# Attention rounds 9 to 17 woven into two expert steps, on one core

## Chip, cores and metric

The kernel runs on one core of a Trainium2 chip. The metric is the device time in microseconds (us) of one execution. Every comparison is with the kernel before.

## What is computed

```python
# attention in chunks of 64 tokens, 8 heads of 64, 2304 tokens in all
scores = scale * np.matmul(q_c, k_c.transpose(0, 1, 2, 4, 3))
scores = scores - np.max(scores, axis=-1, keepdims=True)
attn = np.exp(scores)
attn = attn / (np.sum(attn, axis=-1, keepdims=True) + 1e-09)
x = np.matmul(attn, v_c)                       # -> (2304, 512)
# mixture of 8 experts, each 512 -> 1024 -> 512
P = np.exp(x @ w_gate - max)                   # then 8 rounds of row and column scaling
out += P[:, e:e + 1] * (np.maximum(x @ w1[e], 0.0) @ w2[e])
# one dense layer, 512 -> 2048 -> 512, with elu between
y = elu(out @ w_in) @ w_out
```

Matrix products are done in three passes: each operand is split into a high part (rounded) and a low part (the rest), and high·high, low·high and high·low are added.

## The kernel before

**Tokens.** The 2304 tokens are 18 tiles of 128. Six blocks of three tiles form three *pairs* (p = 0, 1, 2) of 768 tokens. The attention visits the tiles pair by pair, one tile in each of 18 *rounds*, so pair 0 is complete after round 5, pair 1 after round 11, pair 2 after round 17.

**A round** `i` of the attention, on the engines: TensorE forms the scores (`scores_of`, L442, 32 recorded matmuls of 64 rows); VectorE takes the row maximum (L956) and subtracts it (L961); ScalarE does the exponential (L692); VectorE sums the row (L967), adds eps (L969) and takes the reciprocal (L973); GpSimd multiplies (`norm`, L311); TensorE transposes the probabilities (`turn_prob`, L453), ScalarE copies them out of PSUM (`e_copy`, L698), TensorE multiplies them with the values (`values_of`, L468), ScalarE copies the result to `x` (`x_copy`, L703). TensorE's order in round `i` is `scores_of(i)`, `turn_prob(i-3)`, `values_of(i-4)`. The value tile `v_wide` holds 64 rows of values and 64 rows of zeros for each half, so that a matmul can contract over all 128 rows. VectorE writes the zeros at the start.

**A step** `n` is one pair of tokens against one group of 256 hidden columns. It has seven *products* M1 to M7 of six matmuls of 384 columns each (`product`, L477; a scheme of Strassen's kind with 7 products for 8), and a *down* phase of 36 matmuls of 512 columns (L494 to L509) into the accumulators. There are 3 steps for each group, 32 groups of experts (steps 0 to 95) and 8 of the dense layer (steps 96 to 119, kind `elu`). Between a product and the down phase lie a copy on ScalarE (`fork`), an add on VectorE (`join`, L1009), the activation on ScalarE (`high`) and its low part on VectorE (`low`, L1014).

**The operands of the products** come from `x`: four sums on VectorE (`x_sums`, L991), seven high parts on ScalarE (`x_high`, L720), and seven low parts, on GpSimd (`x_low`, L364) or VectorE (L1002). Before a pair's first step TensorE waits for all of them at once (`x_split`).

**Order around the change.** Every engine runs a list written out by hand; semaphores join the lists. TensorE does rounds 0 to 17, then step 0 with what is left of the attention between its products, then the gate of the router for blocks 0 and 1 (`gate_of`, L582), step 1, more gates, step 2. From step 3 on the steps follow without a gap. SyncE issues all loads, in order, from one queue (`load_qk` of 512 KB and `load_v` of two times 128 KB for each round; four buffers each). A load waits for its buffer: `load_qk(i)` for the scores of round i-4, `load_v(i)` for the values of round i-4. What stands behind a waiting load waits too.

Steps 95 to 98 carry the second change of operands: the accumulators of the experts are transposed into `x`, and the operands for the dense layer are formed pair by pair.

## Time and profile before

| | |
|---|---|
| median of 3 runs | 1996.67 us (1993.13 to 1996.77) |
| the profiled execution's own time | 1995.51 us |
| its span in the trace | 1993.7 us |
| TensorE matmul busy | 1945.5 us, 98% |
| VectorE, ScalarE, GpSimd busy | 56%, 36%, 27% |
| mean granted TensorE clock | 0.993 |

The profile is one execution. Busy time of TensorE is a share of the span in which a matmul was in flight. The granted clock is 1.00 for 2.4 GHz and 0.50 for 1.2 GHz. Times in the trace count from the start of the span.

### The profile page before, as it was taken

The page shows a single profiled execution, that of the slowest core. Times are in us where ns is not written, and L with a number is a line of the kernel's source. Part 1 is how long each engine was busy: PE and PEld are TensorE (multiplying, and loading weights), DVE is VectorE, ACT ScalarE, POOL GpSimd, SP SyncE. Part 2 cuts the span into 40 slices and gives each one's busy share as a digit, 9 for nine tenths or more (in the row PEclk, how much of TensorE's full clock was granted, in tenths as well). Part 3 has the DMA queues.
Part 4 walks back from the last instruction along what each step waited for, and adds up shares of the span by engine and source line. Part 5 has one row for each costly group of instructions (what it writes and reads, how often), then busy time and mean ns, then how long its engine had stood idle before and what let it go on. Part 6 is the DMA issues. An engine that isn't in the chain of part 4 may idle for free.

```text
span 1993.7 us, 31492 instructions
## 1 busy us (share of the span) xinstructions
PE 1945.5 (98%) x10738; PEld 1751.2 (88%) x10738; DVE 1123.3 (56%) x1866; ACT 719.5 (36%) x1516; POOL 532.8 (27%) x600
## 2 busy tenths in 40 slices
PE   6799999999999999999999999999999989999999
PEld 5699999988999889998899988999889868998888
DVE  7766654555545555455554555555555576666666
ACT  4532223222233323232223322223323455555554
POOL 5732252222222222222222222222222342222220
PEclk9999999999999999999999999999999989999999
DMA  8110000000000000000000000000000000000002
GB/s 257 52 39 26 22 21 22 21 21 21 21 21 21 21 21 32 31 21 21 21 21 21 21 21 21 21 21 21 21 25 28 11 21 22 21 21 21 21 21 95
DMA packets 20154, 61.40 MB, mean 31 GB/s; under 512 B 2960, under 2 KB 2960, under 8 KB 20112
## 3 DMA queue, kind: packets, MB, share of 16 engines
q1 hardware_dynamic: 20112, 60.84, 9.0%
q8 instruction: 26, 0.43, 0.1%
q14 instruction: 16, 0.13, 0.0%
HBM read 56.12 MB, written 4.72 MB: 31 GB/s over the span
## 4 chain that ended last, share of the span: by engine, by line
PE 93%; DVE 4%; ACT 1%; issue 0%; POOL 0%; ACTq 0%
PE bank L477 44%; PE bank L507 5%; PE bank L494 5%; PE bank L495 5%; PE bank L509 5%; PE bank L508 5%; PE bank L499 5%; PE last_banks L507 3%; PE last_banks L509 3%; PE last_banks L508 3%; PE last_banks L494 3%; PE last_banks L495 3%; PE last_banks L499 3%; DVE x_sum L991 1%; ACT x_hi L720 1%
## 5 line engine op out<-in xcount | busy, mean ns | idle before, releaser
L477 PE MATMUL bank<-x_hi,w_hi 128*128 128x384 f32 x1680 | 568.5, 338 | 14.5 <-DVE x_lo L1002 6.9
L477 PE MATMUL bank<-x_hi,w_lo 128*128 128x384 f32 x1680 | 565.9, 337 | 0.0
L477 PE MATMUL bank<-x_lo,w_hi 128*128 128x384 f32 x1680 | 564.6, 336 | 0.0
L746 ACT ACTIVATE h_raw<-bank 128x384 f32<-128x384 f32 x360 | 176.6, 491 | 746.5 <-PE bank L477 744.7
L1009 DVE TENSOR_TENSOR h_raw<-bank,h_raw 128x384 f32<-128x384 f32 x360 | 200.7, 558 | 421.2 <-PE bank L477 419.6
L477 PEld LDWEIGHTS bank<-x_hi,w_hi 128*128 128x128 f32 x1680 | 316.6, 188 | 24.9 <-issue 7.8
L477 PEld LDWEIGHTS bank<-x_lo,w_hi 128*128 128x128 f32 x1680 | 316.6, 188 | 5.5
L319 POOL TENSOR_TENSOR w_sum<-raw 128x256 f32<-128x256 f32 x40 | 29.5, 739 | 1088.6 <-PE bank L477 1081.7
L477 PEld LDWEIGHTS bank<-x_hi,w_lo 128*128 128x128 f32 x1680 | 316.4, 188 | 0.0
L1027 DVE SCALAR_TENSOR_TENSOR acc<-bank,route,acc 128x512 f32<-128x512 f32 x336 | 240.4, 751 | 125.4 <-PE bank L509 125.4
L755 ACT ACTIVATE h_hi<-h_raw 128x384 fp32r<-128x384 f32 x288 | 151.2, 526 | 208.6 <-DVE h_raw L1009 208.6
L1027 DVE SCALAR_TENSOR_TENSOR acc<-last_banks,route,acc 128x512 f32<-128x512 f32 x168 | 120.2, 751 | 161.8 <-PE last_banks L509 161.8
L507 PE MATMUL bank<-w_hi,h_hi 128*128 128x512 f32 x480 | 188.4, 393 | 3.6 <-DVE h_lo L1014 3.6
L494 PE MATMUL bank<-w_hi,h_hi 128*128 128x512 f32 x480 | 189.3, 394 | 0.7 <-DVE acc L1021 0.7
L1014 DVE SCALAR_TENSOR_TENSOR h_lo<-h_raw,h_hi 128x384 fp32r<-128x384 f32 x288 | 179.8, 625 | 16.1 <-ACT h_hi L755 4.6
L495 PE MATMUL bank<-w_lo,h_hi 128*128 128x512 f32 x480 | 188.5, 393 | 0.0
L509 PE MATMUL bank<-w_hi,h_lo 128*128 128x512 f32 x480 | 187.5, 391 | 0.0
L508 PE MATMUL bank<-w_lo,h_hi 128*128 128x512 f32 x480 | 187.4, 390 | 0.0
L499 PE MATMUL bank<-w_hi,h_lo 128*128 128x512 f32 x480 | 149.2, 392 | 0.0
L347 POOL TENSOR_TENSOR w_lo<-raw,w_hi 128x512 fp32r<-128x512 f32 x80 | 103.8, 1303 | 46.6 <-ACT w_hi L736 44.9
L341 POOL TENSOR_TENSOR w_lo<-w_sum,w_hi 128x256 fp32r<-128x256 f32 x160 | 114.8, 739 | 0.0
L507 PEld LDWEIGHTS bank<-w_hi,h_hi 128*128 128x128 f32 x480 | 90.2, 188 | 25.4 <-DVE h_lo L1014 4.9
(103 smaller groups left out, 2561.0 us busy)
## 6 DMA issues: line engine op xcount, KB each, us to landing
raw<-in_w_up SPq DMA_DIRECT2D x40, 512.0 KB, 3.2
raw<-in_w_down SPq DMA_DIRECT2D x40, 512.0 KB, 3.3
qk<-in_q_k SPq DMA_DIRECT2D x18, 512.0 KB, 5.9
v_wide<-in_v SPq DMA_DIRECT2D x36, 128.0 KB, 3.6
out<-acc SPq DMA_DIRECT2D x18, 256.0 KB, 2.0
gate_w<-in_w_gate SPq DMA_DIRECT2D x1, 16.0 KB, 7.1
```

What stands on the lines that cost most here:

```text
L477: mm = nc.tensor.matmul(up_ps[s], w[:, s, kk, :], xs[:, s, kk, :], start=first and s in (M1, M2, M5), stop=kk == 1 and w is w1_lo, skip_gr ...
L494: nc.tensor.matmul(y_ps[i], h_hi[:, fi, ti, js], w2_hi[:, f, :], start=True, stop=False)
L495: nc.tensor.matmul(y_ps[i], h_hi[:, fi, ti, js], w2_lo[:, f, :], start=False, stop=False)
L499: nc.tensor.matmul(y_ps[TPB * h[1] + j], h_lo[:, fi, ti, js], w2_hi[:, f, :], start=False, stop=False)
L507: nc.tensor.matmul(y_ps[i], h_hi[:, fi, ti, js], w2_hi[:, f, :], start=False, stop=False)
L508: nc.tensor.matmul(y_ps[i], h_hi[:, fi, ti, js], w2_lo[:, f, :], start=False, stop=False)
L509: nc.tensor.matmul(y_ps[i], h_lo[:, fi, ti, js], w2_hi[:, f, :], start=False, stop=True)\
L746: nc.scalar.activation(h_raw[:, to[0], to[1], :], src, ACT.Copy).then_inc(fork_done, 1)
L755: nc.scalar.activation(h_hi[:, h[0], h[1], :], src, ACT.Relu).then_inc(h_hi_done, 1)
L1009: nc.vector.tensor_tensor(raw, src, raw, ALU.add).then_inc(join_done, 1)
L1014: nc.vector.scalar_tensor_tensor(h_lo[:, h[0], h[1], :], src, 0.0, h_hi[:, h[0], h[1], :].bitcast(F32), ALU.max, ALU.subtract).then_inc(h_ ...
L1027: nc.vector.scalar_tensor_tensor(acc[:, t, :], y_ps[i], route_flat[:, bass.ds(EXPERTS * t + expert, 1)], acc[:, t, :], ALU.mult, ALU.add). ...
```

## The change

1. The values tile has 64 rows per head half and no zeros; a values matmul contracts over 64 rows (`v_rows`). One load of 256 KB replaces two of 128 KB. The eight zero fills are gone.
2. `soft` has a 65th column that holds eps, so that the row sum includes it; the add of eps is gone. `norm` writes another tile, `prob`. Both have three buffers.
3. Rounds 0 to 8 use two sets of score banks in turn. Steps 0 and 1 are no longer behind the attention: round 9 goes with M1 of step 0, 10 with M2, and so on to round 14 with M7; rounds 15 to 17 and the last transposes and values go with the products of step 1. The values follow the transpose by one product, not by a round.
4. Low parts of the token sums of pairs 0 and 1 (M5, M6, M3, M7) are formed on VectorE, of pair 2 M6, M3, M7.
5. TensorE waits for the low part of each product before that product (`x_split(u, s)`), in the later pairs too.
6. SyncE's list of loads is written in another order; the loads of the first weights come earlier.
7. The gates, the conversion of the first weights, the scaling rounds of the router (one step later) and `scale_acc` move to fit.

```diff
-OVERLAP = {M1: 18, M5: 19, M3: 20, M7: 21}
-LOWS_POOL = [7, 14, 17, 22, 27, 32]
-LOWS_DVE = [0, 0, 4, 6, 8, 10]
+EARLY = 9
+ROUND_OF = {0: {M1: 9, M2: 10, M5: 11, M6: 12, M3: 13, M7: 14}, 1: {M2: 15, M5: 16, M6: 17, M3: 18, M7: 19, M4: 20}}
+LOWS_POOL = [[M1, M2, M4], [M1, M2, M4], [M1, M5, M2, M4]] + [[M1, M2, M4, M5, M7]] * 3
+LOWS_DVE = [[M5, M6, M3, M7], [M5, M6, M3, M7], [M6, M3, M7]] + [[M6, M3]] * 3
...
             load_qk(0)
             load_qk(1)
+            sp.dma_start(raw1[:, :, :], w_up[0, :, :, :]).then_inc(raw1_loaded, 16)
+            load_qk(2)
             load_v(0)
-            load_qk(2)
+            load_qk(3)
             load_v(1)
-            load_qk(3)
+            sp.dma_start(raw2[:, :, :], w_down[0, :, :, :]).then_inc(raw2_loaded, 16)
             load_v(2)
             load_v(3)
-            for i in range(TILES):
-                if i + DEPTH < TILES:
-                    load_qk(i + DEPTH)
-                if DEPTH <= i:
-                    load_v(i)
-                if i == 1:
+            for i in range(DEPTH, TILES):
+                load_qk(i)
+                load_v(i)
+                if i == 8:
                     sp.dma_start(gate_w[:, :, :], w_gate.rearrange("(k p) e -> p k e", p=P)).then_inc(gate_loaded, 16)
-                    sp.dma_start(raw1[:, :, :], w_up[0, :, :, :]).then_inc(raw1_loaded, 16)
-                    sp.dma_start(raw2[:, :, :], w_down[0, :, :, :]).then_inc(raw2_loaded, 16)
...
-            def x_split(u):
-                pe.wait_ge(x_lo_done, LOWS_POOL[u])
-                if LOWS_DVE[u] > 0:
-                    pe.wait_ge(x_lo_rest, LOWS_DVE[u])
+            def x_split(u, s):
+                if s in LOWS_POOL[u]:
+                    pe.wait_ge(x_lo_done, low_count(LOWS_POOL, u, s))
+                else:
+                    pe.wait_ge(x_lo_rest, low_count(LOWS_DVE, u, s))
...
+            for i in range(EARLY):
+                scores_of(i)
+                if i >= TURN_LAG:
+                    turn_prob(i - TURN_LAG)
+                if i > TURN_LAG:
+                    values_of(i - TURN_LAG - 1)
...
+                def ahead(s):
+                    i = ROUND_OF[n].get(s)
+                    if i is None:
+                        return
+                    if i < TILES:
+                        if n == 1:
+                            pe.wait_ge(acc_done, 5)
+                        scores_of(i)
+                    if i == EARLY:
+                        values_of(i - TURN_LAG - 1)
+                    turn_prob(i - TURN_LAG)
...
+                    i = ROUND_OF[n].get(s)
+                    if i is not None:
+                        if n == 1:
+                            pe.wait_ge(acc_done, 6)
+                        values_of(i - TURN_LAG)
...
-                dve.wait_ge(sum_done, 3 * i + 1)
-                nc.vector.tensor_scalar(row_den[:, :], row_sum[:, :], EPS, None, ALU.add).then_inc(sum_done, 1)
```

**Place one: SyncE's queue, the loads of rounds 4 to 7.** `qk_74` to `qk_77` are the four q and k buffers (rounds 4 to 7 reuse them in turn), `v_wide_78` to `v_wide_81` and `v_rows_78` to `v_rows_81` those of the values. Before, with the q and k of rounds 6 to 8 first and then the values of round 4:

```order
L260 DMA qk_76<-in_q_k 128x1024 [waits scores_done]
L260 DMA qk_77<-in_q_k 128x1024 [waits scores_done]
L260 DMA qk_74<-in_q_k 128x1024 [waits scores_done]
L268 DMA v_wide_78<-in_v 64x512 [waits values_done]
L268 DMA v_wide_78<-in_v 64x512
L260 DMA qk_75<-in_q_k 128x1024 [waits scores_done]
```

The same place in the change:

```order
L279 DMA v_rows_81<-in_v 128x512
L273 DMA qk_74<-in_q_k 128x1024 [waits scores_done]
L279 DMA v_rows_78<-in_v 128x512 [waits values_done]
L273 DMA qk_75<-in_q_k 128x1024 [waits scores_done]
L279 DMA v_rows_79<-in_v 128x512 [waits values_done]
L273 DMA qk_76<-in_q_k 128x1024 [waits scores_done]
```

Before, four loads of q and k (rounds 5 to 8) stood ahead of the first load that waits for values; now only that of round 4 does, and each later one stands behind the values load of the round before it.

**Place two: TensorE, round 5 of the change.** `first_banks` and `last_banks` are the two sets of score banks, `e_t` the transposed probabilities.

```order
L471 MATMUL first_banks<-qk_75 64x64 [waits soft_done,qk_loaded1]
L471 MATMUL first_banks<-qk_75 64x64 x15
L482 MATMUL bank<-ident,prob_87 128x128 [waits prob_done,e_t_done]
L482 MATMUL bank<-ident,prob_87 128x128 x3
L495 MATMUL bank<-e_t,v_rows_79 64x64 [waits e_t_done,v_loaded1]
L495 MATMUL bank<-e_t,v_rows_79 64x64 x15
L471 MATMUL last_banks<-qk_76 64x64 [waits soft_done,qk_loaded2]
```

The order within a round is that of before, with other names: the values of round 1 come behind the scores of round 5 and ahead of those of round 6.

**Place three: GpSimd, around the last low part of pair 0.** `x_lo_51` holds the low parts of pair 0, `x_lo_54` those of pair 1. Before, behind the sixth `norm` from the start of pair 0's low parts:

```order
L364 TENSOR_TENSOR x_lo_51<-x,x_hi_49 128x768 [waits x_hi_done]
L311 TENSOR_TENSOR soft_82<-soft_82,row_rec_97 128x512 [waits sum_done]
L364 TENSOR_TENSOR x_lo_51<-x,x_hi_49 128x768 [waits x_hi_done]
L311 TENSOR_TENSOR soft_83<-soft_83,row_rec_98 128x512 [waits sum_done]
L364 TENSOR_TENSOR x_lo_51<-x_sum_50,x_hi_49 128x768 [waits x_sum_done,x_hi_done]
```

In the change:

```order
L321 TENSOR_TENSOR prob_85<-soft_82,row_rec_98 128x512 [waits e_turned,sum_done]
L321 TENSOR_TENSOR prob_86<-soft_83,row_rec_99 128x512 [waits e_turned,sum_done]
L374 TENSOR_TENSOR x_lo_51<-x,x_hi_49 128x768 [waits x_hi_done]
L374 TENSOR_TENSOR x_lo_54<-x,x_hi_52 128x768 [waits x_hi_done]
L321 TENSOR_TENSOR prob_87<-soft_84,row_rec_98 128x512 [waits e_turned,sum_done]
```

GpSimd's low part of M4 of pair 0 (the first of the two `x_lo` rows) now stands behind the `norm` of round 13; before, one low part followed each `norm`.

## Rows read from the trace of the kernel before

**Rows 1.** Busy time by stretch, then granted clock, DMA share, GB/s.
```profile
0.00:10.00 10.00, 2.26 (x64) 1.92 (x64) 6.53 (x12) 1.91 (x2) 0.85 (x7) 1.00 0.84 265
10.00:20.00 10.00, 7.53 (x168) 6.35 (x168) 8.13 (x19) 3.49 (x6) 3.63 (x4) 1.00 1.05 352
71.72:98.17 26.45, 24.94 (x218) 21.21 (x218) 13.72 (x14) 13.55 (x23) 14.98 (x8) 0.90 0.01 2
98.17:141.57 43.40, 41.98 (x224) 37.86 (x224) 27.60 (x49) 15.12 (x32) 13.71 (x12) 1.00 0.07 25
141.57:157.29 15.72, 15.72 (x82) 14.29 (x81) 10.12 (x22) 4.58 (x10) 5.95 (x7) 1.00 0.20 68
1627.50:1633.30 5.80, 5.74 (x18) 5.77 (x19) 2.21 (x3) 1.01 (x2) 0.00 (x0) 0.50 0.00 0
```

**Rows 2.** TensorE in order of time, rounds 7 to 9.
```profile
30.47 1.12 PE L453 MATMUL bank<-ident,soft 128*128 128x128 f32 x4 [3.89 <-ACT e_t L698]
31.51 1.98 PE L468 MATMUL bank<-e_t,v_wide 128*64 128x64 f32 x32
33.42 1.13 PE L442 MATMUL last_banks<-qk 64*64 64x64 f32 x32
35.72 1.23 PE L468 MATMUL bank<-e_t,v_wide 128*64 128x64 f32 x32
36.88 0.69 PE L442 MATMUL last_banks<-qk 64*64 64x64 f32 x32
38.14 0.66 PE L453 MATMUL bank<-ident,soft 128*128 128x128 f32 x4 [0.56 <-ACT e_t L698]
```

**Rows 3.** SyncE's queue in order of time: start, duration of the issue.
```profile
36.99 1.10 SPq L268 DMA_DIRECT2D v_wide<-in_v  x2
```

**Rows 4.** Loads from issue to landing (last column), issued at 38.1 and 145.2.
```profile
qk<-in_q_k SPq DMA_DIRECT2D x1, 512.0 KB, 4.1
raw<-in_w_up SPq DMA_DIRECT2D x1, 512.0 KB, 3.3
```

**Rows 5.** VectorE in order of time, one round and one sum.
```profile
58.02 0.64 DVE L956 TENSOR_REDUCE row_max<-last_banks 128x8 f32<-128x512 f32 x1
58.69 0.69 DVE L961 TENSOR_TENSOR soft<-last_banks,row_max 128x512 f32<-128x512 f32 x1
59.30 0.68 DVE L967 TENSOR_REDUCE row_sum<-soft 128x8 f32<-128x512 f32 x1
60.01 1.02 DVE L969 TENSOR_SCALAR row_den<-row_sum 128x8 f32<-128x8 f32 x1
61.06 0.20 DVE L973 RECIPROCAL row_rec<-row_den 128x8 f32<-128x8 f32 x1
68.11 0.91 DVE L991 TENSOR_TENSOR x_sum<-x_sum,x 128x768 f32<-128x768 f32 x1
70.10 2.39 DVE L991 TENSOR_TENSOR x_sum<-x 128x768 f32<-128x768 f32 x1
```

**Rows 6.** GpSimd in order of time, the same stretches.
```profile
58.18 1.04 POOL L311 TENSOR_TENSOR soft<-soft,row_rec 128x512 f32<-128x512 f32 x1 [0.35 <-DVE row_rec L973]
59.18 1.82 POOL L364 TENSOR_TENSOR x_lo<-x_sum,x_hi 128x768 fp32r<-128x768 f32 x1
```

**Rows 7.** TensorE, VectorE, GpSimd at the entry of step 97, in order of time.
```profile
1627.56 0.66 PE L477 MATMUL bank<-x_hi,w_hi 128*128 128x384 f32 x1 [6.94 <-DVE x_lo L1002]
1622.41 5.01 DVE L1002 TENSOR_TENSOR x_lo<-x_sum,x_hi 128x768 fp32r<-128x768 f32 x2
1619.93 6.67 POOL L364 TENSOR_TENSOR x_lo<-x,x_hi 128x768 fp32r<-128x768 f32 x3 [2.22 <-ACT x_hi L720]
1631.78 0.56 DVE L1009 TENSOR_TENSOR h_raw<-bank,h_raw 128x384 f32<-128x384 f32 x1 [2.63 <-PE bank L477]
1636.55 0.39 PE L494 MATMUL bank<-w_hi,h_hi 128*128 128x512 f32 x1
```

**Rows 8.** The chain of work, two blocks of the gate: start, us.
```profile
122.61 2.80 PE last_banks L582 x16
```

More of the change, by code:

```diff
@@ L78, in nth_hidden, with low_count @@
     return HIDDEN[kind].index(h) + 1
+def low_count(lows, u, s):
+    return sum(len(lows[v]) for v in range(u)) + lows[u].index(s) + 1
 def pair_tile(p, i):
@@ L864, in _ @@
-            relu_step(0, begin=True, after=overlap)
-            for c in range(3, 7):
-                x_high(0, 1, c)
-            for c in range(3):
-                x_high(0, 2, c)
+                    x_high(0, M2)
+            x_copy(5)
+            e_copy(6)
+            exp_of(9)
+            fork(0, up_a, H11, M1, "first")
+            x_copy(6)
+            e_copy(7)
+            x_high(0, M5)
+            exp_of(10)
+            x_copy(7)
+            x_high(0, M6)
+            e_copy(8)
@@ new lines, in _ @@
+            exp_of(11)
+            x_high(0, M3)
+            fork(0, up_b, H22, M5, "first")
+            x_copy(8)
+            e_copy(9)
+            exp_of(12)
+            x_high(0, M7)
+            fork(0, up_a, H12, M6, "first")
+            x_copy(9)
+            high(0, H11, "first")
+            e_copy(10)
+            exp_of(13)
+            x_high(0, M4)
+            x_copy(10)
+            x_high(1, M1)
+            e_copy(11)
+            exp_of(14)
+            x_high(1, M2)
+            x_copy(11)
@@ L869, in _ @@
+            e_copy(12)
+            x_high(1, M3)
+            exp_of(15)
+            x_copy(12)
+            x_high(1, M7)
+            e_copy(13)
+            exp_of(16)
+            fork(1, up_b, H22, M5, "first")
+            x_copy(13)
+            high(1, H11, "first")
+            x_high(1, M4)
+            e_copy(14)
+            exp_of(17)
+            fork(1, up_a, H12, M6, "first")
+            x_copy(14)
+            e_copy(15)
+            x_copy(15)
             gate_copy(0)
             gate_copy(1)
[L872 to L878 removed]
@@ L1129, in _ @@
[L1129 to L1146 removed]
+            softmax_head(0)
@@ new lines, in _ @@
+            join(0, H11, up_c, M2, 1, "first")
+            softmax_head(13)
+            x_low(0, M7)
+            softmax_tail(12)
+            low(0, H11, "first")
+            softmax_head(14)
+            softmax_tail(13)
+            join(0, H12, up_b, M3, 3, "first")
+            join(0, H22, up_a, M7, 2, "first")
+            low(0, H12, "first")
+            low(0, H22, "first")
+            low(0, H21, "first")
+            softmax_tail(14)
+            x_sums(1, (M5,))
+            for i in range(TPB):
+                add_tile(0, 0, i, "first")
@@ new lines, in _ @@
+            x_sums(1, (M6,))
+            for i in range(TPB, 2 * TPB):
+                add_tile(0, 0, i, "first")
+            x_low(1, M5)
+            x_sums(1, (M3,))
+            softmax_head(15)
+            x_low(1, M6)
+            x_sums(1, (M7,))
+            softmax_head(16)
+            x_low(1, M3)
+            softmax_tail(15)
+            join(1, H11, up_c, M2, 1, "first")
+            softmax_head(17)
+            x_low(1, M7)
+            softmax_tail(16)
+            low(1, H11, "first")
@@ new lines, in _ @@
+            softmax_tail(17)
+            join(1, H12, up_b, M3, 3, "first")
+            join(1, H22, up_a, M7, 2, "first")
+            low(1, H12, "first")
+            low(1, H22, "first")
+            logits_of(0)
+            logits_of(1)
+            low(1, H21, "first")
+            x_sums(2, (M5, M6))
+            for i in range(TPB):
+                add_tile(1, 1, i, "first")
+            x_sums(2, (M3, M7))
+            for i in range(TPB, 2 * TPB):
+                add_tile(1, 1, i, "first")
```

517 lines of the change are left out of this document (265 added, 252 removed).

## The prediction, made before the changed kernel had run

> **What bounds the kernel now.** I read the busy time by stretch first [rows 1]. From 141.57 us, where step 3 begins, TensorE is busy without a gap: step 3 takes 15.72 us, all of it matmul, and the later steps are like it. So the change can move the time in two places only: ahead of step 3, and at the entry of the dense layer (steps 96 to 98), where the trace has TensorE's one long wait behind the start, 6.94 us [rows 7]. The time ahead of step 3 is what I work out, since everything behind it follows TensorE's work.
>
> Ahead of step 3 the attention runs almost alone until 71.72 us. Scores of round 9 start at 36.88 us [rows 2]; from there VectorE sets the pace, with 3.2 us or more for a round: in the one shown row maximum, subtraction, row sum, add of eps and reciprocal start at 58.02, 58.69, 59.30, 60.01 and 61.06 [rows 5]. The add of 8 numbers took 1.02 us because GpSimd held something VectorE needed: its low part ran from 59.18 for 1.82 us, to 61.00, where the add ends [rows 6]. Step 0 with its rest of the attention took 26.45 us (71.72 to 98.17), steps 1 and 2 with all gates 43.40 us, of which TensorE was busy 41.98 [rows 1].
>
> **The start, rounds 0 to 4.** VectorE loses the zero fills and the adds; scores are ahead by a second bank set. That is worth little, since loads set the pace. Ahead of the q and k of round 4 stand, in the new list, four of 0.524 MB, two weights of 0.524 MB and four values of 0.262 MB; with its own bytes 4.72 MB. The first 10 us brought 265 GB/s, the next 10 us 352 [rows 1]: 2.65 MB by 10 us and the other 2.07 MB in 5.9 us, so round 4 starts at 15.9 us (14.5 if 352 held from about 1 us, 17.8 at 265 throughout). Before, these bytes were fewer by the two weights, which came behind.
>
> **Rounds 5 to 9: a wait that the new list makes.** This is the heart of the forecast. TensorE's round i is scores(i), transpose(i-3), values(i-4), as before. `load_v(i)` waits for values(i-4), the end of round i. In the new list the q and k of round i+1 stand behind `load_v(i)`, so they are only asked for when round i is over, though their buffer has been free since round i-3. Scores(i+1) need them, and each round then costs its own TensorE time plus a whole load. Before, rounds 5 to 8 had their q and k asked for ahead of any values load, and that lead was kept.
>
> The load's price, D: the values load takes one issue, half of the 1.10 us that two took [rows 3], so 0.55; then q and k land. With the queue otherwise idle 512 KB took 3.3 us; behind a pair of value loads q and k took 4.1 [rows 4]. I take 3.65, the middle, since one load in front is half the issues and the same bytes: D = 4.2 us; bounds 3.85 and, with the old pair's 1.10 us of issue and 4.1, 5.2.
>
> TensorE's part: scores took 0.69 us at the upper clock and 1.13 at the lower, the transpose 0.66 (1.12), the values of 128 rows 1.98 at the lower [rows 2]. The new values matmuls have the scores' form, 64 rows by 64 columns, so I give them the scores' time. Which clock? After an idle time of 3.89 us the transpose took 1.12 us and the clock stayed low up to the values at 35.72, five microseconds of work later [rows 2]. With 4.2 us idle in each round and at most 3.4 us of work, I take the lower level for all of rounds 4 to 8: 1.13 + 1.05 + 1.13 = 3.3 us (the transpose at its start-to-start time, 30.47 to 31.51). At the upper level it would be 0.67 + 0.6 + 0.67 = 1.95.
>
> The Trainium skill, page "TensorE: Matmul & The Clock Gate", section "HAM oscillation — how this bites in real kernels", describes this pattern: when the work between two waits for loads is short against the wait, the array goes back to 1.2 GHz in every turn of the loop. By that rule the sum stays as it is; without it, it would be 1.35 us less in each of five rounds. The trace shows one such gap only, and agrees.
>
> So rounds 4 to 8 take 3.3 + 4.2 = 7.5 us each and round 9 starts at 15.9 + 5 x 7.5 = **53.4 us, 16.5 later than before**.
>
> **Round 9 to the end of step 0.** Round 9 does scores and values(5) first; q and k of round 10 land 1.1 + 1.1 + 4.2 later, at 59.8. Round 9 goes on with transpose, M1 and values(6). M1 is six matmuls; at the lower clock 18 took 5.8 us [rows 1], so 1.9 us; the round is over at 53.4 + 1.1 + 1.1 + 1.05 + 1.9 + 1.0 = 59.6, and round 11 can start 4.2 us later, at 63.8. From here the loads are one round ahead: a round can't take less than D = 4.2 us. TensorE needs 3.0 of it. VectorE needs, per round, maximum and subtraction 0.67 + 0.61 + about 0.1, row sum and reciprocal 0.71 + 0.15, and one token sum and one low part at 0.91 each [rows 5]: 4.1. The two are level, so I take 4.2 with the product's lows just in time. Round 14 starts at 63.8 + 3 x 4.2 = 76.4.
>
> M4 then waits for a chain, since GpSimd does its low part behind the `norm` of round 13, and VectorE does the tail of round 13 behind the head of round 14: scores(14) to 77.1, VectorE behind by 1.5 (it is as loaded as the loads), head 1.4, tail 0.9, `norm` 1.04, low part 1.82 [rows 6] = 83.8. TensorE has had no work since about 79.4, falls to the lower clock, and does M4 in 1.9. The down phase is 15.72 less seven products of 1.05, 8.4 us, plus 1.6 for its first part at the lower clock. Step 0 ends at 95.7; before it ended at 98.2. The interleaving has bought back 14 of the 16.5 us.
>
> **Steps 1 and 2.** Work of before in this stretch: two steps of 15.72, three pairs of gate blocks of 2.80 [rows 8] and 1.5 for their small transposes = 41.3 us. New in it: three scores of 0.69, six transposes of 0.6 and six values of 0.67 = 9.7. I add 5.5 us of waits: 3 for VectorE in rounds 15 to 17 (4.1 against TensorE's 3.0 each), 1 for the accumulators' last adds, which must leave the banks ahead of scores(15), 0.6 for the last copy of `x` ahead of the down phase, 1 for the low parts of the second weights, which now stand behind the maximum over all partitions. Bounds 2 and 10. Step 3 starts at 95.7 + 41.3 + 9.7 + 5.5 = 152.2 us against 141.57: **+10.6 us**.
>
> **The entry of the dense layer.** TensorE stood still up to 1627.56 us for VectorE's last low parts of pair 1 [rows 7]. With a wait per product M1, M2 and M5 go at 1620.6, since GpSimd's lows of pair 1 stand ahead of the three of pair 2 that began at 1619.93. M6 and M3 still wait for VectorE's two lows, which took 5.01 us from 1622.41, held up by those three (6.67 us). So the wait moves from M1 to M3; what is late next is the activation of H11: VectorE's add for it ran at 1631.78 behind 2.63 us of idle time, so it can start at 1629.15, and five operations of about 0.55 (add, negated part, exponential, elu, high part) end at 1632.0. The first down matmul ran at 1636.55. **Gain 4.5 us**; 4.3 after a little more of lower clock. Bounds 2.6 (only those 2.63 us) and 6.9.
>
> Steps 3 to 95 lose nothing that I see: the scaling of the router starts one step later with the same work, and `scale_acc` meets adds that come 8 us after it could begin.
>
> **Sum.** +10.6 - 4.3 = +6.3 us on the profiled execution's 1995.5: 2001.8. Its time lies 1.2 below the median of before, 1996.67; I set the forecast between the two, at **2002.5 us**, +0.3%.
>
> **Rivals.**
> 1. *Same wait, upper clock* (0.15). If the clock doesn't fall in rounds 4 to 9, 5 x 1.35 + 1.3 = 8 us go: 1994.5. Against it stands the 3.89 us gap.
> 2. *The change does what it says* (0.10), the other side. If q and k come at VectorE's pace instead of waiting for values, rounds 4 to 8 take 0.786 MB / 352 GB/s = 2.2 us each, round 9 starts at 27.1, and the time is 26 us lower, about 1976. It decides below D = 3.3 us, where gain and loss are level (6.3 us in seven loads); a load of 512 KB alone took 3.3 [rows 4], so it takes an order of loads other than the one I read.
> 3. *VectorE and GpSimd in each other's way* (0.18). VectorE now does 7 more low parts in the rounds in which GpSimd has its `norm`. A token sum took 0.91 us in one place and 2.39 in another [rows 5]. If each of 23 sums and lows waits 0.35 us more, +8: 2010.
>    The Trainium skill, page "Advanced Engine Details and Errata", section "Mode Summary", notes that VectorE's second SBUF port is shared with GpSimd and that the two block each other. It speaks against the move of lows to VectorE; the pair 0.91 and 2.39 agrees, but other reasons for the 2.39 are not excluded.
> 4. *No gain at the dense layer, the rest as forecast* (0.05): 2006.5.
>
> The forecast has 0.52. Slower is 0.6: nearly all of it, and rivals 3 and 4. A measurement of this kernel can tell about 0.2% (4 us) from no change. Faster by more is 0.18 (rival 2, a third of rival 1, a little of stalls over-counted), same 0.22. D at its bounds moves the sum by -2 and +9, the waits of steps 1 and 2 by -3.5 and +4.5, the start by -1.4 and +1.9. The range is 1992 to 2012.
>
> **What would show it.** SyncE: each q and k load of rounds 5 to 10 is issued within 0.6 us behind a values load, which is issued at the end of a round; TensorE's waits ahead of scores name the q and k load, about 3.5 us or more each, five times. Scores(5) to (8) about 7.5 us apart, each 1.1 us long. Scores(9) near 53. M4 of step 0 waits for GpSimd's low part. Step 3 starts near 152. At step 97 the 6.94 us are gone from M1 and about 1.5 to 3 us stand ahead of M3 and the first down matmul. I am wrong if scores(9) come before 45 us, if the five rounds run at 0.69 us per scores, or if rounds 10 to 14 take over 5 us.

## The result, and the profile after

| | before | after |
|---|---|---|
| median | 1995.49 us (4 runs, 1993.13 to 1996.77) | 2016.74 us (4 runs, 2016.67 to 2018.26) |
| span in the trace | 1993.7 us | 2014.9 us |
| TensorE matmul busy | 1945.5 us | 1950.5 us |
| mean granted clock | 0.993 | 0.989 |

The ratio is 1.011, 95% interval 1.0092 to 1.0127. The direction was forecast. The size was not: the forecast was 2002.5 us, with a range of 1992 to 2012.

The busy time by stretch comes first, as in [rows 1]: length, busy time and number of instructions of TensorE matmul, weight load, VectorE, ScalarE, GpSimd, then granted clock, DMA share and GB/s.

```profile
0.00:56.64 56.64, 25.67 (x472) 21.45 (x472) 18.64 (x34) 16.82 (x32) 22.84 (x33) 0.84 0.41 154
56.64:97.13 40.49, 33.22 (x519) 29.14 (x520) 32.75 (x48) 20.32 (x37) 16.33 (x14) 0.93 0.42 138
155.24:163.98 8.74, 0.00 (x2) 0.03 (x1) 0.89 (x3) 0.63 (x1) 1.24 (x3) 0.67 0.00 0
163.98:181.62 17.64, 17.64 (x78) 16.20 (x79) 6.84 (x12) 3.77 (x8) 6.48 (x8) 0.87 0.18 60
```

Round 9 starts at 56.64 us, step 0 ends at 97.13, step 2 ends at 155.24, and then TensorE does nothing for 8.74 us. Step 3 takes 17.64 us, partly at the lower clock, where it took 15.72. Up to round 9 the DMA engines were busy only 41% of the time: the loads are late because they are asked for late, not because the engines are full.

SyncE's queue, rounds 6 to 8. The number behind the start is the time that the issue took.

```profile
35.92 0.33 SPq L279 DMA_DIRECT2D v_rows<-in_v  x1
36.29 0.43 SPq L273 DMA_DIRECT2D qk<-in_q_k  x1
44.05 0.33 SPq L279 DMA_DIRECT2D v_rows<-in_v  x1
44.42 0.43 SPq L273 DMA_DIRECT2D qk<-in_q_k  x1
51.96 0.33 SPq L279 DMA_DIRECT2D v_rows<-in_v  x1
52.33 0.68 SPq L295 DMA_DIRECT2D gate_w<-in_w_gate  x1
53.06 0.50 SPq L273 DMA_DIRECT2D qk<-in_q_k  x1
```

TensorE in the same rounds, which answers to [rows 2]; in brackets the idle time and what ended it.

```profile
39.93 1.14 PE L471 MATMUL first_banks<-qk 64*64 64x64 f32 x32 [4.05 <-DMA qk<-in_q_k]
40.99 1.11 PE L482 MATMUL bank<-ident,prob 128*128 128x128 f32 x4
42.04 1.97 PE L495 MATMUL bank<-e_t,v_rows 64*64 64x64 f32 x32
47.84 1.13 PE L471 MATMUL last_banks<-qk 64*64 64x64 f32 x32 [3.83 <-DMA qk<-in_q_k]
...
56.64 1.13 PE L471 MATMUL last_banks<-qk 64*64 64x64 f32 x32 [4.72 <-DMA qk<-in_q_k]
```

Read the two together. Values end at 44.0, both loads are issued at 44.05 and 44.42, q and k let the scores go at 47.84. So each round holds a whole load in which TensorE waits.

TensorE's waits over the whole execution: total, times, longest.

```profile
PE last_banks L471 <- DMA qk<-in_q_k: 25.4, 8, 4.7
PE first_banks L471 <- DMA qk<-in_q_k: 8.9, 3, 4.1
PE first_banks L504 <- POOL w_lo L351: 8.7, 1, 8.7
PE first_banks L504 <- ACT h_raw L800: 7.3, 3, 4.3
PE first_banks L504 <- POOL x_lo L374: 2.6, 1, 2.6
```

The third row is the one that the forecast has not. This is GpSimd ahead of it:

```profile
147.46 0.74 POOL L329 TENSOR_TENSOR w_sum<-raw 128x256 f32<-128x256 f32 x1 [9.61 <-DMA raw<-in_w_up]
...
149.67 0.74 POOL L343 TENSOR_TENSOR w_sum<-raw,w_sum 128x256 f32<-128x256 f32 x1
155.90 0.38 POOL L438 PARTITION_ALL_REDUCE small<-small  x1 [5.50 <-issue]
163.12 1.40 POOL L351 TENSOR_TENSOR w_lo<-raw,w_hi 128x256 fp32r<-128x256 f32 x2 [6.84 <-issue]
```

A 0.38 us maximum over the partitions stands between the sums and the low parts of the second weights. It has 5.50 us in front and 6.84 behind in which GpSimd waits for nothing that the profile shows: VectorE's part of the maximum was done at 148.65, and from 150.41 to 163.12 the DMA engines moved nothing. The profile's page calls spans of custom instructions on GpSimd rough, so part of this time may belong to the operation itself. The sums themselves start late: the load of those weights waits for gates 4 and 5, which went behind M7 of step 2, and it was issued at 144.29 us (before the change at 125.44).

Step 97, the counterpart of [rows 7]: two rows of TensorE, then ScalarE, then VectorE.

```profile
1648.46 0.41 PE L504 MATMUL first_banks<-x_hi,w_hi 128*128 128x384 f32 x1 [1.38 <-DVE x_lo L1098]
1654.00 0.69 PE L504 MATMUL first_banks<-x_hi,w_hi 128*128 128x384 f32 x1 [4.26 <-ACT h_raw L800]
1653.05 0.52 ACT L837 ACTIVATE h_exp<-h_raw 128x384 f32<-128x384 f32 x1 [7.53 <-DVE h_raw L1105]
1653.48 0.47 ACT L800 ACTIVATE h_raw<-first_banks 128x384 f32<-128x384 f32 x1
1645.69 5.12 DVE L1098 TENSOR_TENSOR x_lo<-x_sum,x_hi 128x768 fp32r<-128x768 f32 x2
1652.47 0.54 DVE L1105 TENSOR_TENSOR h_raw<-bank,h_raw 128x384 f32<-128x384 f32 x1
```

M1 no longer waits. M6 waits 1.38 us for its low part, and M3 4.26 us for ScalarE's copy out of PSUM at 1653.48. That copy (L800) stands in ScalarE's list behind the negated part of H11 (L837), which had to wait for VectorE's add at 1652.47, and the add stood behind two low parts and two sums.

### The profile page after: what moved, and what is told of

Read it like the earlier page. It is cut to its first block, busy times and chain, and to the rows that moved or that the text cites. A ratio compares the mean times of both kernels' runs of the same rounds, so it can differ in the third digit from the quotient of the medians.

```text
span 2014.9 us, 31518 instructions
## 1 busy us (share of the span) xinstructions
PE 1950.5 (97%) x10738; PEld 1756.9 (87%) x10738; DVE 1116.5 (55%) x1847; ACT 716.9 (36%) x1516; POOL 520.3 (26%) x596
## 4 chain that ended last, share of the span: by engine, by line
PE 91%; issue 3%; DVE 2%; DMA 2%; POOL 1%; ACT 1%; SPq 0%; POOLq 0%; DVEq 0%
PE first_banks L504 37%; PE bank L504 6%; PE bank L521 5%; PE bank L522 5%; PE bank L526 5%; PE bank L534 5%; PE bank L535 5%; PE bank L536 5%; PE last_banks L534 3%; PE last_banks L535 3%; PE last_banks L536 3%; PE last_banks L522 3%; PE last_banks L526 3%; PE last_banks L521 3%; DMA qk<-in_q_k 2%
## 5 line engine op out<-in xcount | busy, mean ns | idle before, releaser
L504 PE MATMUL first_banks<-x_hi,w_hi 128*128 128x384 f32 x1440 | 489.6, 340 | 20.0 <-POOL w_lo L351 8.7
L504 PE MATMUL first_banks<-x_hi,w_lo 128*128 128x384 f32 x1440 | 486.2, 338 | 0.0
L504 PE MATMUL first_banks<-x_lo,w_hi 128*128 128x384 f32 x1440 | 485.2, 337 | 0.0
L800 ACT ACTIVATE h_raw<-first_banks 128x384 f32<-128x384 f32 x360 | 176.5, 490 | 742.7 <-PE first_banks L504 741.0
L1105 DVE TENSOR_TENSOR h_raw<-first_banks,h_raw 128x384 f32<-128x384 f32 x240 | 133.7, 557 | 387.7 <-PE first_banks L504 387.2
L504 PEld LDWEIGHTS first_banks<-x_hi,w_hi 128*128 128x128 f32 x1440 | 272.1, 189 | 30.5 <-issue 13.5
L504 PEld LDWEIGHTS first_banks<-x_lo,w_hi 128*128 128x128 f32 x1440 | 272.3, 189 | 5.6
L504 PEld LDWEIGHTS first_banks<-x_hi,w_lo 128*128 128x128 f32 x1440 | 271.9, 189 | 0.0
```

Of the source, the lines that this page charges most:

```text
L504: mm = nc.tensor.matmul(up_ps[s], w[:, s, kk, :], xs[:, s, kk, :], start=first and s in (M1, M2, M5), stop=kk == 1 and w is w1_lo, skip_gr ...
L800: nc.scalar.activation(h_raw[:, to[0], to[1], :], src, ACT.Copy).then_inc(fork_done, 1)
L1105: nc.vector.tensor_tensor(raw, src, raw, ALU.add).then_inc(join_done, 1)
```

## Experiments on the changed kernel, one part at a time

Times below are medians. The kernel before was run beside every experiment, at 1994.8 to 1996.5 us. Since its median moves by 1 to 2 us from one such group to the next, small differences are given with the place in the trace where they arise. The start of step 3 is the first TensorE row of that step, which in the kernel before is at 141.41 us ([rows 1] cut their stretch one row later).

**One: the order of loads.**

```diff
-            for i in range(DEPTH, TILES):
-                load_qk(i)
-                load_v(i)
+            for i in range(TILES):
+                if i + DEPTH < TILES:
+                    load_qk(i + DEPTH)
+                if i >= DEPTH:
+                    load_v(i)
```

> The changed kernel with one edit: SyncE's list asks for the q and k of round i+4 ahead of the values of round i, as before the change; where the weights stand in the list is left. Theory (the order of loads costs the time): TensorE's waits of about 4 us for q and k in rounds 5 to 9 are gone or under 1 us, scores(9) start between 27 and 37 us where they start at 56.64 now, and step 3 starts 16 to 24 us earlier, so that the time is 1993 to 2001 us against 2016.7. Rival A (VectorE and GpSimd set the pace from round 9 on): scores(9) come early all the same, but rounds 9 to 14 take over 5 us each, step 0 ends less than 10 us earlier and the time stays above 2007. Rival B (the lower clock and the matmuls' own time make the rounds slow): scores(9) still start after 45 us.

Measured: 1986.62 us, ratio to before 0.9958 (0.9942 to 0.9975). TensorE, rounds 7 and 9 of this kernel (some of the 32 matmuls of a group stand in rows of their own, left out here):

```profile
24.85 0.64 PE L473 MATMUL first_banks<-qk 64*64 64x64 f32 x30
25.78 0.65 PE L484 MATMUL bank<-ident,prob 128*128 128x128 f32 x4 [0.29 <-ACT e_t L752]
26.36 1.08 PE L497 MATMUL bank<-e_t,v_rows 64*64 64x64 f32 x29
...
30.17 0.69 PE L473 MATMUL last_banks<-qk 64*64 64x64 f32 x32
```

The waits for q and k of rounds 5 to 9 are gone, and a round takes 2.5 us, held by ScalarE's copy (0.29) and TensorE itself at the upper clock. Scores(9) start 26.5 us earlier, and step 3 at 132.98 us, 31.0 earlier. That is more than I expected: another 2.3 us come back between scores(9) and scores(15) (39.23 us for 41.48) and 2.3 from there to step 3, since in these stretches too loads had been late (waits of 1.66 and 1.67 us in the changed kernel). With this line alone mended, the change is 9 us faster than the kernel before.

**Two: where the maximum over partitions stands.** On GpSimd, with the negation and the exponential that need it moved into and behind step 3:

```diff
             w1_sums(1, 2, "relu")
-            pool.wait_ge(part_max_done, 1)
-            nc.gpsimd.partition_all_reduce(...)
             w1_lows(1)
             w2_lows(1)
+            pool.wait_ge(part_max_done, 1)
+            nc.gpsimd.partition_all_reduce(...)
```

> The changed kernel with the maximum over all partitions on GpSimd moved behind the low parts of the second weights (its negation on VectorE and the router's exponential on ScalarE follow it by as much, into and behind step 3). Theory (step 3 waits 8.7 us for GpSimd because that maximum, with about 5.5 us ahead of it and 6.8 us behind it, stands in front of the low parts): the wait ahead of step 3 is under 1.5 us, step 3 starts near 155.5 us instead of 163.98 and takes about 16 us instead of 17.8, the time is 2005 to 2009 us. Rival (the late load of the second weights sets the start of step 3, whatever stands behind it): the wait shrinks by no more than 4 us and the time stays above 2011.

Measured: 2005.80 us, 10.9 below the changed kernel. GpSimd here:

```profile
149.90 0.74 POOL L343 TENSOR_TENSOR w_sum<-raw,w_sum 128x256 f32<-128x256 f32 x1
150.72 1.44 POOL L351 TENSOR_TENSOR w_lo<-raw,w_hi 128x256 fp32r<-128x256 f32 x2
...
164.72 0.38 POOL L440 PARTITION_ALL_REDUCE small<-small  x1 [6.58 <-issue]
```

The low parts follow the sums at once, step 3 starts at 155.16 us without a wait and takes 15.5. The late load of the weights is then hidden; the rival falls. Of the 10.9 us, 8.8 are the wait and the rest is step 3 at the upper clock.

The other order, the maximum ahead of the sums as it was before the change:

```diff
-            w1_sums(1, 2, "relu")
             pool.wait_ge(part_max_done, 1)
             nc.gpsimd.partition_all_reduce(...)
+            w1_sums(1, 2, "relu")
```

> The changed kernel with the maximum over all partitions on GpSimd ahead of the sums of the second weights, as before the change. Theory (the 5.5 us ahead of it are GpSimd fetching another program for the operation, and pass unseen if GpSimd stands idle in front of it): the maximum starts near 150 us instead of 155.9, the sums 6.8 us behind it, step 3 starts 2 to 4 us earlier, time 2012 to 2015 us. Rival (those microseconds are paid after the wait, wherever it stands): the maximum starts at 155 us again, the sums are now behind it too, and step 3 starts 2 to 4 us later, time 2018 to 2021 us.

Measured: 2012.49 us, step 3 at 159.14 instead of 163.98, 4.8 us earlier where I expected 2 to 4.

```profile
147.56 0.38 POOL L437 PARTITION_ALL_REDUCE small<-small  x1 [10.13 <-DVE small L1295]
155.31 0.71 POOL L329 TENSOR_TENSOR w_sum<-raw 128x256 f32<-128x256 f32 x1 [7.37 <-issue]
```

With 10.13 us of idle time ahead of it, the maximum starts 0.14 us after VectorE has released it (147.42); the 5.5 us in front are not seen. The 7.37 us behind stay. In all ten runs in which the next operation had its inputs, 6.8 to 7.4 us lie behind the maximum; in experiment two GpSimd then waits for TensorE anyway, and they cost nothing. In front there are 5.5 to 6.6 us unless GpSimd is idle there. I took this for the fetching of program code, but no run shows what it is: in the changed kernel the DMA engines moved nothing from 150.41 to 163.12.

**Three: ScalarE's list in step 97.** Both copies out of PSUM ahead of the negated part:

```diff
                 fork(n, up_a, H11, M1, "elu")
+                fork(n, up_b, H22, M5, "elu")
+                fork(n, up_a, H12, M6, "elu")
                 neg(n, H11)
-                fork(n, up_b, H22, M5, "elu")
                 exp_neg(n, H11)
-                fork(n, up_a, H12, M6, "elu")
```

> The changed kernel with ScalarE's list of step 97 alone in another order: the two copies of products out of PSUM (H22 and H12) stand ahead of the negated part of H11, which waits for VectorE's add. Theory (TensorE's 4.26 us ahead of M3 of step 97 come from ScalarE standing at the negated part, 7.53 us idle, while the copies that TensorE needs are behind it): the 4.26 us are under 1 us, the lower clock behind them is gone, and the first down matmul comes 2 to 5 us earlier; time 2012 to 2015 us. Rival (VectorE's sums and low parts ahead of its add for H11 set the down phase, whoever copies): TensorE's wait moves behind M4 and gives back under 1 us, time 2016 to 2017 us.

Measured: 2014.13 us, 2.6 lower. TensorE in step 97:

```profile
1648.42 0.41 PE L504 MATMUL first_banks<-x_hi,w_hi 128*128 128x384 f32 x1 [1.41 <-DVE x_lo L1103]
1650.92 0.41 PE L504 MATMUL first_banks<-x_hi,w_hi 128*128 128x384 f32 x1 [1.22 <-DVE x_lo L1103]
1655.39 0.47 PE L521 MATMUL bank<-w_hi,h_hi 128*128 128x512 f32 x1 [2.14 <-ACT h_hi L848]
```

The 4.26 us ahead of M3 are now 1.22, for VectorE's low part, and 2.14 us wait behind M7, for the high part of H11. The first down matmul comes 2.6 us earlier (1658.01 to 1655.39). One of this kernel's four runs took 2019.2 us; the place in the trace speaks for the 2.6. Both theories hold a part: ScalarE's order cost 2.6 us, and VectorE's queue ahead of the add keeps the 2.14. The version with all orders mended, below, moves two sums out of that queue, and the 2.14 us are gone there; but its M3 and M7 ran at the lower clock, so that its first down matmul comes 3.97 us behind the start of M3 where it was 4.47.

**Four: the clock in the waits.** 20 transposes more in each of rounds 4 to 8, into an unused bank:

```diff
                     values_of(i - TURN_LAG - 1)
+                    for _ in range(20):
+                        nc.tensor.transpose(bank[2][:, 0:P], ident[:, :], ident[:, :])
```

> The changed kernel with 20 more 128x128 transposes of the identity into an unused bank behind the values matmuls of each of rounds 4 to 8, so that TensorE is busy through most of its wait for q and k; no result is touched. Theory (TensorE's own part of those rounds is at the lower clock because it idles 4 us in each): scores take 0.69 us instead of 1.13 and values 1.15 instead of 1.97, a round falls from 7.98 to 6.2 to 6.8 us, scores(9) start at 49 to 52 us instead of 56.64, time 2008 to 2013 us. Rival (the clock is low for another reason): the rounds stay at 8 us or grow by what the transposes overrun the wait, scores(9) at 56 us or later, time 2016 or more.

Measured: 2013.42 us, scores(9) at 53.05.

```profile
31.71 0.69 PE L471 MATMUL last_banks<-qk 64*64 64x64 f32 x32 [1.71 <-DMA qk<-in_q_k]
32.34 0.66 PE L482 MATMUL bank<-ident,prob 128*128 128x128 f32 x4
32.93 1.15 PE L495 MATMUL bank<-e_t,v_rows 64*64 64x64 f32 x32
34.01 2.40 PE L654 MATMUL bank<-ident 128*128 128x128 f32 x20
```

Work that does nothing makes the kernel faster. The engine is busy through most of the wait, so from round 5 on scores take 0.69 us instead of 1.13, the transpose 0.66 instead of 1.11, values 1.15 instead of 1.97. Rounds 5 and 6 take 6.4 and 6.5 us. Rounds 4, 7 and 8 take 9.3, 7.4 and 7.5, since there q and k let the next scores go only 5.0 to 5.2 us after the values load was issued, for 4.0 in the other two; this is why 3.6 us were gained up to scores(9) and not 5 to 8, and why they were later in these rounds was not tried. That the lower clock comes with the idle time is shown. By the Trainium skill, page "TensorE: Matmul & The Clock Gate", section "HAM oscillation — how this bites in real kernels", a loop of short work and long waits is throttled in each turn; the trace agrees, with scores of 1.13 us in each of the five rounds and of 0.69 once the waits are filled.

**Five: the eight low parts back on GpSimd**, on top of the mended order of loads. Edit: `LOWS_POOL[0]` and `[1]` take all seven, `LOWS_DVE[0]` and `[1]` none, and the calls move from VectorE's list to GpSimd's, between the `norm` of the same rounds.

> The changed kernel with q and k asked for ahead of the values (1986.6 us), and with the eight low parts of pairs 0 and 1 that the change gave to VectorE back on GpSimd, between the normalisations of the same rounds. Theory (in rounds 9 to 14 VectorE is what paces, 3.4 to 4.5 us a round; the port that both use costs little): with GpSimd at 1.04 + 1.82 us a round and VectorE relieved of 0.91 the six rounds take 0 to 3 us less, step 0 ends 0 to 3 us earlier, time 1984 to 1987 us. Rival (GpSimd's normalisation then stands behind a low part and reaches TensorE late): rounds 9 to 14 take 2 to 6 us more, 1989 to 1993 us.

Measured: 1984.38 us, and step 3 at 130.51 instead of 132.98. So this part of the change costs some 2 us; ranges of the two kernels touch (1983.75 to 1985.39, 1985.26 to 1988.64), the place in the trace speaks for it. The trace does not bear out the theory that VectorE's relief shortens rounds 9 to 14: scores(14) start at 50.81 us, and at 50.78 without this edit. The gain arises behind them. M4 of step 0 starts 0.4 us earlier (56.93 for 57.35), and M4 and the start of the down phase run at the upper clock where they had fallen to the lower one, so that scores(15) start 2.0 us earlier (67.40 for 69.40). The edit was not meant to touch the clock, so about 1.6 of the 2 us are luck.

The third rival can be read from the changed kernel's own trace. In rounds 9 to 17 VectorE's eight low parts took 0.95 or 0.96 us each, and its eight sums 0.91 to 0.96 but for one of 1.81: no sign of 0.35 us more for each. With the low parts back on GpSimd six of the eight sums took 1.42 to 2.48 us. So the two engines do slow each other (in the changed kernel GpSimd's `norm` took up to 1.65 us for 1.04), but VectorE's own operations were slowed less with the low parts on VectorE.

## Experiments on the kernel before

**The wait per product alone**, in steps 96 to 98 (u is the pair's index, 3 to 5):

```diff
+                    if x_ready is not None and x_ready >= PAIRS:
+                        x_split_of(x_ready, s)
                     product(n, p, s)
...
-                if x_ready is not None:
+                if x_ready is not None and x_ready < PAIRS:
                     x_split(x_ready)
```

> The kernel before with one edit: in steps 96 to 98 TensorE waits for the low parts of each product instead of all seven. Theory (the wait per product moves the stall from M1 to M6, M3 and, through ScalarE's order, to the down phase): TensorE's 6.94 us ahead of M1 of step 97 are gone, 1.4 us stand ahead of M6 and about 4.3 ahead of M3, and the time is 1 to 3 us lower, 1993 to 1995 us. Rival (as the prediction had it): 4.5 us lower, 1991. Rival (nothing): 1995.5.

Measured: 1993.84 us, ratio 0.9993 (0.9984 to 1.0003), which can't be told from nothing. The trace gives the size: from the closing matmul of step 96 (L507) to the end of the span 373.3 us, where it was 375.4; 2.1 us won. TensorE:

```profile
1628.20 0.41 PE L477 MATMUL bank<-x_hi,w_hi 128*128 128x384 f32 x1 [1.38 <-DVE x_lo L1011]
1633.75 0.69 PE L477 MATMUL bank<-x_hi,w_hi 128*128 128x384 f32 x1 [4.25 <-ACT h_raw L755]
```

The 6.94 us ahead of M1 [rows 7] have turned into 1.38 and 4.25, the same pair as in the changed kernel.

**Values of 64 rows alone**, with one load in place of two and no zero fills:

```diff
-                pe.wait_ge(v_loaded[j], 32 * (i // DEPTH + 1))
-                if i < DEPTH:
-                    pe.wait_ge(zeroed, 2 * i + 2)
+                pe.wait_ge(v_loaded[j], 16 * (i // DEPTH + 1))
...
-                            mm = nc.tensor.matmul(x_ps[i % 2][HD * g:HD * g + HD, m, cs], v_wide[j][:, g, m, c, :],
-                                                  e_t[:, m, cs], start=True, stop=True)
+                            mm = nc.tensor.matmul(x_ps[i % 2][rows, m, cs], v_rows[j][rows, m, c, :], e_t[rows, m, cs],
+                                                  start=True, stop=True)
```

> The kernel before with one edit: values of 64 rows (one load of 256 KB for a tile instead of two halves into a zero-filled tile, no zero fills, matmuls 64 rows by 64 columns). Theory (a values matmul costs TensorE the same with 64 rows as with 128, 1.15 us for the 32 at the upper clock, and in the attention VectorE and the loads set the pace): the values rows show 1.15 and 1.97 us as with 128 rows, the start gains at most the zero fills and one issue a round, time 1992.5 to 1996 us against 1995. Rival (the prediction's assumption): they take the scores' 0.69 and 1.13 us and the time is 2 to 4 us lower.

Measured: 1995.12 us, ratio 0.9995 (0.9986 to 1.0005). The groups by form: busy us and mean ns of one matmul stand behind the bar. First the kernel before, 128 rows, then this one:

```profile
L468 PE MATMUL bank<-e_t,v_wide 128*64 128x64 f32 x576 | 22.9, 238 | 0.0
```

```profile
L464 PE MATMUL bank<-e_t,v_rows 64*64 64x64 f32 x576 | 22.7, 234 | 0.0
```

Half the rows, the same time. At the upper clock 32 of the old ones took 1.15 us, as the new ones do:

```profile
38.73 1.15 PE L468 MATMUL bank<-e_t,v_wide 128*64 128x64 f32 x32
```

I had given these matmuls the time of the scores, which have the same form and 255 ns each in this view too; but 32 scores take 0.69 us and 32 values 1.15. The form of a tile is not enough to price a group: the two differ in how their matmuls follow each other, and why was not tried.

**The new order of loads alone**, in the kernel before:

```diff
-            for i in range(TILES):
-                if i + DEPTH < TILES:
-                    load_qk(i + DEPTH)
-                if DEPTH <= i:
-                    load_v(i)
-                if i == 1:
+            for i in range(DEPTH, TILES):
+                load_qk(i)
+                load_v(i)
+                if i == 5:
```

> The kernel before with one edit: SyncE's list asks for q and k of round i+1 behind the values of round i, as the change does; gate and first weights stand behind the values of round 5. Theory (the order alone makes a wait of a whole load in each round that has no other work, in any schedule): rounds 5 to 17 take 7.5 to 8.5 us each, with two value loads' issues perhaps 9, where they took 2.5 to 4, step 0 starts at 115 to 135 us instead of 71.72, the time is 2040 to 2060 us. Rival (the cost of 31 us in the changed kernel comes from the order together with its interleaving and its weights loaded early): the time is below 2025 us.

Measured: 2067.55 us, ratio 1.0361 (1.0344 to 1.0378). TensorE's waits:

```profile
PE last_banks L440 <- DMA qk<-in_q_k: 71.9, 14, 8.5
```

14 waits, most of some 5 us, rounds of 8.7 to 9.4 us (scores at 99.47, 108.82, 118.05), and step 0 at 143.38 instead of 71.72. The cost is above the range that I expected: the rounds are about as long as the longest that I had allowed, and round 5 took 12.6 us, since in this list the loads of the gate and of the first two weights stand ahead of the next q and k (the wait of 8.5 us). So about 3.7 of the 72 us belong to where those three loads stand. All 13 rounds from 5 to 17 pay; the interleaving of the changed kernel hides most of it from round 10 on. Nothing else of the change is needed to make the wait.

## The change with its orders mended

Orders one, two and three together; VectorE's last two sums of pair 2 also go behind the add and the elu of H11 in step 97.

> The three edits together: q and k asked for ahead of the values, the maximum over partitions behind the low parts of the second weights, ScalarE's copies of step 97 ahead of the negated part; in addition VectorE's last two token sums of pair 2 stand behind the add and the elu of H11 of step 97 instead of ahead of them. Theory (they act in three places, and what one gives the others leave): 1986.6 less 10.9 (what the second edit gave alone) less 2.6 (the third alone) less about 1.5 for the sums, 1970 to 1974 us. Rival (with the loads early again the second edit's wait is hidden or turns up elsewhere, and the gains overlap): above 1977.

Measured: 1971.79 us, ratio 0.9884 (0.9868 to 0.9901). Step 3 starts at 123.97 us: 40.0 earlier than in the changed kernel, where one gave 31.0 and two 8.8. They act in different places and add up.

Then, on top of it, the eight low parts on GpSimd and the low part of M4 ahead of `norm(13)`:

> The version with three orders mended (1971.8 us), with the eight low parts of pairs 0 and 1 back on GpSimd and the low part of M4 of pair 0 ahead of the normalisation of round 13. Theory: the low parts give 2.2 us as they did with only q and k ahead, the 3.0 us that M4 of step 0 waits for GpSimd fall to about 1; 1967 to 1970 us. Rival (VectorE's add for H22 releases M4 at the same moment, and the low parts overlap with it): 1970 to 1972.

Measured: **1968.93 us**, ratio 0.9864 (0.9848 to 0.9881), step 3 at 119.98. M4 waits 0.5 us for VectorE's add where it waited 3.0 for GpSimd, and scores(15) start at 65.67 instead of 69.75: 2.6 us come from M4's start, 1.5 from M4 and the down phase at the upper clock. This is the fastest version by its median; its range (1967.97 to 1969.91) overlaps that of the next one.

Or, with the low part of M4 moved as above but the eight low parts left on VectorE, the first weights loaded later:

> The version with three orders mended (1971.8 us), with the first weights' loads behind q and k of round 4 and of round 9 instead of among the first four, their sums, high and low parts that much later on GpSimd and ScalarE, and the low part of M4 of pair 0 ahead of the normalisation of round 13. Theory (the 1.05 MB of weights hold up q and k of rounds 2 to 4, TensorE's waits of 2.7, 0.8 and 2.6 us, and rounds 5 to 8 have room for them): round 4 starts 2 to 3 us earlier, time 1967 to 1970 us. Rival (ScalarE paces rounds 5 to 8, and the seven high parts that now fall there, some 0.4 us each, take it all back): 1971 to 1974.

Measured: 1970.46 us (1968.74 to 1971.23), between the other two and between what theory and rival had. Round 4 starts at 14.64 instead of 16.57 us, but scores(9) only 0.7 us earlier (29.67 for 30.37). The rival's reason is not borne out: the lead is still 2.0 us at scores(8) (25.91 for 27.88), with two of the four groups of high parts on ScalarE done by then. The 1.3 us are lost in round 8 alone, 0.86 of them in the middle of its values, where TensorE waits for nothing that the profile shows.

## Why the prediction was wrong

The ledger from the traces, in us. The first four rows are times and lengths, the last three how much later (+) than before that point comes:

| place | forecast | measured |
|---|---|---|
| round 4 starts | 15.9 | 15.88 |
| rounds 4 to 8 | 5 x 7.5 = 37.5 | 40.76 (15.88 to 56.64) |
| round 9 to the end of step 0 | 42.3 | 40.49 |
| steps 1 and 2 | 56.5 | 66.85, of which 8.74 the wait ahead of step 3 |
| step 3 starts (before: 141.41) | +10.6 | +22.6 |
| step 4 starts (157.12, after 181.62) | +10.6 | +24.5 |
| the end | +6.3 | +21.2 |

- **The heart held.** q and k behind a values load that waits for the end of the round: D was put at 4.2 us, and issue to scores took 4.0 (35.92 to 39.93), 3.8 (44.05 to 47.84) and, with the gate's load between, 4.7. The experiments on the order of loads show it alone: it is worth 31.0 us in the changed kernel and 72 in the one before.
- **The clock held in the rounds, not at M4.** Scores of 1.13 us and transposes of 1.11 in all five rounds; filling the waits brings them back to the upper level. At M4 of step 0 the forecast had the lower clock too and counted 2.5 us for it; there the wait was 2.6 us and the granted clock stayed at 1.00 (80.00 to 97.13). That is why round 9 to the end of step 0 took 1.8 us less than forecast, although round 14 came 5.2 us late.
- **Mis-sized: values at the scores' 1.13 us.** They took 1.97 (1.67 in one of the five rounds), and 1.15 at the upper clock where 0.67 was put. In the five rounds TensorE was busy 20.09 us and not 16.5, and it waited 20.7 and not 21.0: that is the miss of 3.3 us up to round 9.
- **M4 waits for GpSimd's low part**, as forecast: 2.6 us idle, start at 87.65 instead of 83.8, on a round 9 that was 3.2 late.
- **The step that failed: the term of the waits in steps 1 and 2, "1 for the low parts of the second weights, which now stand behind the maximum over all partitions".** I saw the order and put 1 us on it without a row for the price. The wait was 8.74 us, and step 3 took 1.9 more at the lower clock behind it: 9.7 of the 14.9 us that the sum missed. The trace of before has a good part of the price: there the same maximum has 22.10 us of idle time in front and 6.84 us of unexplained time between it and the sums of the weights.

```profile
129.20 0.38 POOL L410 PARTITION_ALL_REDUCE small<-small  x1 [22.10 <-DVE small L1160]
136.42 0.73 POOL L319 TENSOR_TENSOR w_sum<-raw 128x256 f32<-128x256 f32 x1 [6.84 <-issue]
```

I had not read that gap, because it lay under TensorE's work. The 5.50 us in front could not be read there, since the idle time hides them. Moving it into a chain that TensorE waits for made it count. Experiment two shows it: with the maximum behind the low parts all of it comes back, 8.8 us at the start of step 3 and 10.9 in the time. The term had to be sized with the maximum's surroundings: 12.7 us from the last sum to the first low part.

- **The entry of the dense layer: right in kind, half the size.** 4.3 us forecast, with a lower bound of 2.6; the wait per product alone gives 2.1, and the stretch from step 96 on is 2.1 us shorter in the changed kernel too (373.3 us for 375.4). The wait did move to M3, but I followed VectorE's add and the five operations of H11, and not ScalarE's list, in which TensorE's copies stand behind one of those five. Another 1.2 us were won between steps 4 and 96, which I did not trace.
- **Rival 2, what the interleaving is for, was priced rightly as a part.** Scores(9) at 27.1 if loads come in time; 30.17 measured. With both orders mended step 3 starts 17.4 us ahead of before (123.97). So the net +22.6 us at step 3 is -17.4 for the rest of the change, +31.0 for the order of loads and +9.0 for the maximum (132.98 to 123.97).
- **The third rival did not come**, as the lengths of VectorE's operations show (experiment five).

The rest of the 14.9 us is small: 3.3 up to round 9, 1.8 less in step 0, 2.6 more in steps 1 and 2 beside the failed term, 1.0 too much gain from step 4 on, and 0.2 for where step 3 of before was taken to begin. Steps 1 and 2 took 10.35 us more than forecast: TensorE worked 55.2 us where 51.0 were counted, among them the values at 1.15 us, and waited 11.7 us (8.74 of them for the maximum) where 5.5 were. The upper bound for these waits was 10, so the one term alone nearly filled it.

Some figures of the working do not follow from its own numbers. The four waits of steps 1 and 2 add up to 5.6 and not 5.5, and the middle of 3.3 and 4.1 is 3.7 and not 3.65; neither matters. The remark that the interleaving had bought back 14 of the 16.5 us is wrong by more: a step 0 that ends at 95.7 instead of 98.2 is 2.5 us ahead, so 19 us were bought back, part of it because three rounds of the attention move into step 1. The sum does not use that remark.

## What to carry to other kernels

A queue is read with its waits: ask of each load what stands in front of it in its queue and what that one waits for. In these kernels a load behind another that waits for the end of a round could not be ahead of its round, although it had four buffers, and that cost more (31 us) than the rest of the change gave (17).

When an operation is moved, price it with the unexplained time around it in the trace, not with its own length. Time that is hidden today is part of the price as soon as the operation stands in a chain that someone waits for.

A wait split by product gives no more than the next wait leaves: walk each engine's own list in order behind it, to the next operation that must wait.

## What the runs showed of the hardware

- GpSimd's maximum over all partitions shows 0.38 us in the trace, 6.8 to 7.4 us without visible cause behind it, and 5.5 to 6.6 us in front of it when GpSimd was at work just before; after 10 or 22 us of idle time it starts 0.14 us after its release.
- A values matmul of 64 rows by 64 columns takes the same as one of 128 by 64: 234 and 238 ns in the means, 1.15 us for 32 at the upper clock.
- 20 transposes that nobody uses, placed in each wait of 4 us, brought TensorE to the upper level for the next rounds and made the kernel 3.3 us faster (2016.74 to 2013.42).
- VectorE's sums of 128x768 numbers took 0.91 to 0.96 us in seven of eight cases in the changed kernel; with GpSimd's eight low parts in the same rounds six of eight took 1.42 to 2.48.
